# Routing in groups of three tiles, first-half rows from six tiles, scatters between the key copies, and another order of the last tile

## The reference, cut to what matters

```
attn_out = _attn_ref(q, k, v)                     # band of 31 keys and 24 block summaries per query
x = attn_out.transpose(0, 2, 1, 3).reshape(1536, 512)
logits = x @ w_gate
noisy_logits = logits + log1p(exp(x @ w_noise)) * noise
top2 = the two largest of noisy_logits            # of 8 experts
top2_w = softmax over the two
for e in range(8):
    for k in range(2):
        mask = top2[:, k] == e
        h = maximum(x[mask] @ w1[e], 0)
        out[mask] += top2_w[mask, k] * (h @ w2[e])
h = out @ w_in;  r = maximum(h, 0);  result = (s * r * r + b) @ w_out
```

## Time and profile before

| | us |
|---|---|
| median of 3 runs | 706.74 (703.12, 706.74, 707.35) |
| the profiled execution, its own time | 703.65 |
| its span | 702.0 |
| PE busy in the span | 683.7 |
| DVE, ACT, POOL busy | 261.0, 216.1, 309.4 |

### The profile page before, as it was taken

How to read it: one execution, slowest core, us unless ns; L and a number is a source line. 1 busy time by engine, 2 the same in 40 slices (tenths; PEclk the granted TensorE clock), 3 DMA queues, 4 the chain that set the end, 5 groups by cost and what they waited for, 6 DMA issues and landing times.

```text
span 702.0 us, 10455 instructions
## 1 busy us (share of the span) xinstructions
PE 683.7 (97%) x4065; PEld 569.8 (81%) x4065; DVE 261.0 (37%) x551; ACT 216.1 (31%) x499; POOL 309.4 (44%) x278
## 2 busy tenths in 40 slices
PE   8898989999999999999999999999999999999998
PEld 3466789788888888888999899888888888888886
DVE  6467766431230212312121244944505235051330
ACT  2458955221220311203131313411324113141231
POOL 1415745567988396697889562302021020200000
PEclk9999968999999999999999999999999999999999
DMA  9996433699979195792979599932012020100001
GB/s 261 255 289 183 168 136 134 221 397 362 405 258 400 54 388 197 254 382 76 384 249 397 183 336 315 379 113 61 1 60 61 1 60 1 45 15 1 0 1 60
DMA packets 55966, 132.34 MB, mean 189 GB/s; under 512 B 8712, under 2 KB 11016, under 8 KB 55920
## 3 DMA queue, kind: packets, MB, share of 16 engines
q0 software_dynamic: 28144, 82.77, 33.7%
q1 hardware_dynamic: 27155, 47.77, 20.9%
q10 hardware_dynamic: 621, 1.18, 0.7%
HBM read 104.79 MB, written 25.97 MB: 186 GB/s over the span
## 4 chain that ended last, share of the span: by engine, by line
PE 91%; issue 2%; DMA 2%; ACT 2%; DVE 1%; POOL 1%; SPq 0%; POOLq 0%
PE ps L380 27%; PE ps L382 27%; PE ps L381 27%; PE ps L1531 2%; PE ps L1464 1%; PE ps L1419 1%; DMA v_all<-v_all 1%; PE ps L1447 1%; PE ps L1391 1%; ACT prob L693 1%; PE ps L1427 1%; PE ps L1669 1%; PE ps L1456 1%; POOL kwin L567 1%; POOL x_sorted L582 1%
## 5 line engine op out<-in xcount | busy, mean ns | idle before, releaser
L546 POOL TENSOR_TENSOR w_lo<-w_raw,w_hi 128x1024 fp32r<-128x1024 f32 x56 | 134.2, 2416 | 20.5 <-DMA w_hi<-in_w_pieces_dram 19.7
L967 DVE SCALAR_TENSOR_TENSOR h_lo<-ps,h_hi 128x448 fp32r<-128x448 f32 (+2 forms) x64 | 36.7, 574 | 197.2 <-ACT h_hi L704 197.2
L380 PE MATMUL ps<-x_hi,w_hi 128*128 128x448 f32 (+2 forms) x256 | 88.2, 345 | 0.0
L704 ACT ACTIVATE h_hi<-ps 128x448 fp32r<-128x448 f32 (+2 forms) x64 | 32.3, 505 | 181.0 <-PE ps L382 181.0
L381 PE MATMUL ps<-x_lo,w_hi 128*128 128x448 f32 (+2 forms) x256 | 88.0, 344 | 0.0
L382 PE MATMUL ps<-x_hi,w_lo 128*128 128x448 f32 (+2 forms) x256 | 88.0, 344 | 0.0
L380 PE MATMUL ps<-w_hi,h_hi 128*128 128x512 f32 x216 | 86.8, 402 | 0.0
L382 PE MATMUL ps<-w_hi,h_lo 128*128 128x512 f32 x216 | 84.5, 391 | 0.0
L381 PE MATMUL ps<-w_lo,h_hi 128*128 128x512 f32 x216 | 84.5, 391 | 0.0
L1313 DVE SCALAR_TENSOR_TENSOR sqr<-relu,sbb 128x512 f32<-128x512 f32 x48 | 36.2, 754 | 112.9 <-ACT relu L838 112.2
L381 PE MATMUL ps<-y_lo,w_hi 128*128 128x512 f32 (+1 forms) x200 | 76.1, 381 | 0.0
(11 more groups left out here) (228 smaller groups left out, 1125.0 us busy)
## 6 DMA issues: line engine op xcount, KB each, us to landing
w_raw<-in_w_pieces_dram POOLq DMA_DIRECT2D x56, 512.0 KB, 13.8
w_hi<-in_w_pieces_dram POOLq DMA_DIRECT2D x56, 512.0 KB, 15.3
xb<-x_sorted SPq DMA_DIRECT2D x25, 256.0 KB, 7.5
y_sorted<-ysb SPq DMA_DIRECT2D x25, 256.0 KB, 2.0
x_sorted<-zrow SPq DMA_DIRECT2D x7, 896.0 KB, 15.0
w_raw<-in_w_pieces_dram SPq DMA_DIRECT2D x8, 512.0 KB, 4.7
w_hi<-in_w_in_dram POOLq DMA_DIRECT2D x8, 512.0 KB, 7.8
w_raw<-in_w_in_dram SPq DMA_DIRECT2D x8, 512.0 KB, 8.3
```

What stands on the lines that cost most here:

```text
L380: pe.matmul(acc, l_hi, r_hi, start=start, stop=False, skip_group_check=True)
L546: pool.tensor_tensor(piece(w_lo, slot, k), piece(w_raw, slot, k), piece(w_hi, slot, k).bitcast(F32), ALU.subtract).then_inc(pieces_split, 1)
L704: act.activation(hi[:, i // FT % 2, i % FT, 0:rows], ps[:, i % FT, 0:rows], ACT.Relu).then_inc(sg.hhi_ready, 1)
L967: dve.scalar_tensor_tensor(out=lo[:, at, i % FT, 0:rows], in0=ps[:, i % FT, 0:rows], scalar=0.0, in1=hi[:, at, i % FT, 0:rows].bitcast(F32 ...
```

## The change

`GROUP_OF` becomes four groups of three tiles (was 4, 3, 3, 2), so a group's `noise_exp` and `noise_ln` come in slots 3, 6 and 9 (were 4, 7, 10), and its DVE steps one slot earlier too; the last group has three tiles. All ranks stand in bank 7. `EARLY_TILES` is 6. POOL's first 12 scatters are issued one by one between the last key copies, most of them after a wait for a progress count of PE (`pv_done`: values of so many tiles done; `turned`: twice per tile). The last slot of the loop is written out in another order, and in the first head `ranks(3)` moves into the middle of `down_early(0)`.

```diff
-EARLY_TILES = 7
+EARLY_TILES = 6
-GROUP_OF = ((0, 4), (4, 7), (7, 10), (10, 12))
-RANK_BANK = (7, 7, 2, 7)
+GROUP_OF = ((0, 3), (3, 6), (6, 9), (9, 12))
-ROUND_AT = (8, 9, 11)
-GMAX = 4
+ROUND_AT = (8, 10, 11)
+GMAX = 3
@@ POOL
-            key_windows(9)
-            key_windows(10)
             pool.wait_ge(zeros_done, 16)
             pool.wait_ge(pos_ready, 1)
-            for t in range(*GROUP_OF[0]):
-                if t == 2:
-                    key_windows(11)
-                scatter(t)
-            for g in range(1, len(GROUP_OF)):
+            scatter(0, 0)
+            pool.wait_ge(pv_done, 7)
+            scatter(0, 1)
+            key_windows(9)
+            pool.wait_ge(turned, 16)
+            scatter(1, 0)
+            pool.wait_ge(pv_done, 8)
+            scatter(1, 1)
+            key_windows(10)
+            pool.wait_ge(turned, 18)
+            scatter(2, 0)
+            pool.wait_ge(pv_done, 9)
+            scatter(2, 1)
+            pool.wait_ge(pos_ready, 2)
+            scatter(3, 0)
+            key_windows(11)
+            scatter(3, 1)
+            pool.wait_ge(pv_done, 10)
+            scatter(4, 0)
+            pool.wait_ge(scores_done, 12)
+            scatter(4, 1)
+            pool.wait_ge(turned, 22)
+            scatter(5, 0)
+            pool.wait_ge(pv_done, 11)
+            scatter(5, 1)
+            for g in range(2, len(GROUP_OF)):
@@ ACT, first_head
                 noise_exp(last)
+                noise_ln(last)
                 up_early(0)
-                noise_ln(last)
                 up_early(1)
@@ DVE, the loop and behind it
                 if s == NT - 1:
-                    route_top(2)
-                    route_chosen(2)
+                    normalise(s)
                 if s >= 1:
                     read_logits(s - 1)
+                if s in (3, 6, 9):
+                    route_a(s // 3 - 1)
                 if s in (4, 7, 10):
-                    route_a(s // 3 - 1)
-                if s in (5, 8):
                     route_top(s // 3 - 1)
-                if s == 6:
-                    route_c(0)
-                if s == 9:
-                    route_c(1)
+                if s in (5, 8, 11):
+                    route_c(s // 3 - 1)
+                if s == 8:
                     early_count()
-                normalise(s)
-                if s in (5, 8):
+                if s < NT - 1:
+                    normalise(s)
+                if s in (4, 7, 10):
                     route_chosen(s // 3 - 1)
...
-            route_c(2)
             split_first(1)
             read_logits(NT - 1)
             route_a(3)
             up_early(0)
+            up_early(1)
             split_first(2)
-            up_early(1)
             route_top(3)
@@ PE, the loop and behind it
-            for s in range(1, NT):
+            for s in range(1, NT - 1):
...
-                if s == 6:
+                if s == 5:
                     pe.wait_ge(xT_ready, s)
                     ranks(0)
-                if s == 9:
+                if s == 8:
                     pe.wait_ge(xT_ready, s)
                     ranks(1)
                     early_counts()
                 logits(s - 1)
                 values(s)
+            turn_probs(NT - 1)
+            turn_x(NT - 2)
+            values(NT - 1)
+            pe.wait_ge(xT_ready, NT - 1)
             ranks(2)
+            logits(NT - 2)
@@ PE, first_rows and first_part
+                pe.wait_ge(rank_read, 3)
                 turn_x(NT - 1)
...
-                pe.wait_ge(rank_read, 3)
-                down_early(0)
-                pe.wait_ge(lg_ready, NT)
-                ranks(3)
-                pe.matmul(ps[:, 6, 0:E], ones[:, :], before[:, NT, :], start=True, stop=True).then_inc(counts_done, 1)
+                down_early(0, rank_last)      # rank_last: these three steps, after the first of its two row tiles
```

More of the change, by code:

```diff
@@ L578, in spread_means, with scatter @@
                                    ).then_inc(means_in[b][part], 16)
-            def scatter(t):
-                for c in range(2):
-                    pool.indirect_dma_start(out=x_sorted, out_offset=bass.IndirectOffsetOnAxis(pos_i[:, t, c:c + 1], 0),
-                                            in_=x_sb[:, t, :], in_offset=None).then_inc(scattered, 16)
+            def scatter(t, c):
+                pool.indirect_dma_start(out=x_sorted, out_offset=bass.IndirectOffsetOnAxis(pos_i[:, t, c:c + 1], 0),
+                                        in_=x_sb[:, t, :], in_offset=None).then_inc(scattered, 16)
             key_windows(2)
@@ L606, in _ @@
                 for t in range(*GROUP_OF[g]):
-                    scatter(t)
+                    for c in range(2):
+                        scatter(t, c)
             pool.wait_ge(scores_done, NT)
@@ L1055, in route_c @@
                 dve.wait_ge(rank_done, g + 1)
-                rank = ps[:, RANK_BANK[g], L_RANK:L_RANK + n * E].rearrange("p (t e) -> p t e", e=E)
+                rank = ps[:, 7, L_RANK:L_RANK + n * E].rearrange("p (t e) -> p t e", e=E)
                 dve.tensor_tensor(rank_all[:, at:to, :], rank, bc(cst[:, C_ECAP:C_ECAP + E], n, 1), ALU.add).then_inc(rank_read, 1)
@@ L1477, in ranks @@
                 for t in range(at, to):
-                    acc = ps[:, RANK_BANK[g], L_RANK + (t - at) * E:L_RANK + (t - at + 1) * E]
+                    acc = ps[:, 7, L_RANK + (t - at) * E:L_RANK + (t - at + 1) * E]
                     pe.matmul(acc, tri[:, :], chosen[:, t, :], start=True, stop=False)
@@ L1495, in _ @@
             values(0)
-            for s in range(1, NT):
-                if 3 < s + 1 < NT:
+            for s in range(1, NT - 1):
+                if s >= 3:
                     scores(s + 1)
-                if s == 7:
+                if s == 6:
                     pe.wait_ge(rank_read, 1)
-                if s == 10:
+                if s == 9:
                     pe.wait_ge(half_ready, 1)
@@ L1603, in down_early, with rank_last @@
                     down(head, 0, 0, PART, g, between, ha_hi, ha_lo)
+                def rank_last(t):
+                    if t == 1:
+                        pe.wait_ge(lg_ready, NT)
+                        ranks(3)
+                        pe.matmul(ps[:, 6, 0:E], ones[:, :], before[:, NT, :], start=True, stop=True).then_inc(counts_done, 1)
                 up_early(0)
                 up_early(1)
-                pe.wait_ge(rank_read, 3)
-                down_early(0)
-                pe.wait_ge(lg_ready, NT)
-                ranks(3)
-                pe.matmul(ps[:, 6, 0:E], ones[:, :], before[:, NT, :], start=True, stop=True).then_inc(counts_done, 1)
+                down_early(0, rank_last)
                 up_early(2)
```

## The result

The changed kernel took **709.88 us** (median of 22 runs, 704.42 to 718.75), the kernel before 706.34 us beside it (22 runs, 702.24 to 708.78): ratio 1.0055, 95% interval 1.0034 to 1.0076. Forecast were 709 us and "within 1%", so the number and the class held. The same pair was then timed on two more chips, and there the ratio was not the same: 1.0076 [1.0041, 1.0110] where the kernel before takes 703.99 us, but **0.9954 [0.9930, 0.9978]** where it takes 715.99 us. Both things want an explanation: the +3.5 us, which is the sum of the prediction, and the 12 us by which the kernel before is longer on some chips while the changed one is longer by 4 only, of which the prediction knew nothing.

A forecast was written before the change was run, and what follows sets the result against it. PE bounds the kernel, busy 97% of the span; only the chain to the second rows was open. Loop and last tile +0.4, routing +0.8, scatters +2.5 make 3.7 us, added to 705.2: 709 us, own range 706 to 712.

The forecast's parts named there:

- The loop: Attention loop up to tile 11's last exponentials: earlier routing gains against added table loads, sum -0.5 us, bounds -2.3 and +1.75.
- Single scatters among the key copies: POOL's 12 scatters between key copies in the loop: just hidden, cost 0, or up to 1.5 us.
- T: Start of the first head's first product on PE, forecast 0.4 us later, near 103.7 us.
- The last tile: Last exponentials to the first head's first product, at half clock: 12.2 us, 0.9 more; bounds 0 and +1.5.
- Routing of the last group: DVE's chain in the first head until the last group's row numbers are ready: T + 13.0, 0.8 us later.
- The ranks' wait: PE reaches `ranks(3)` in the first head about 0.6 us ahead of DVE's choices and waits, at no further cost.
- Scatters: Last group's scatters on POOL, six instead of four: 2.5 us more before the second rows load.
- The new wait: PE's wait in the first head for the second 256 rows: grows from 1.35 us to 4.0 us.
- Rival 2: PE's clock falls to half in the longer wait for the second rows, costing 2.8 us: 712 us; chance 0.15.
- Rival 3: The last tile keeps full clock, its PE work takes 5 us less: 701.5 us; chance 0.20.
- The forecast case: Every link of the chain to the second rows as summed: 709 us, range 706 to 712; chance 0.50.

The follow-up runs named there:

- b1: The changed kernel run again, unaltered, on a fast chip: 709.37 us, ratio 1.0076 to the kernel before.
- g2: The changed kernel with the third group's noise logarithm replaced by an exponential, so no table loads in the last slots: 711.50 us, ratio 1.0078 to the kernel before.
- b3: The kernel before with scatters of groups 0 and 1 issued singly, each behind a mark of PE's work: 705.66 us, ratio 1.0009.
- b4: b3 plus a new routing order for the last group: `ranks(3)` inside `down_early(0)`, `route_c(3)` ahead of `split_first(3)`: 705.13 us, ratio 1.0006 to the kernel before.
- g1: b4 plus seven useless products ahead of the last tile's turn and eight in the wait for the second rows: 707.38 us, ratio 1.0025 to the kernel before.
- g3: The changed kernel with tile 10's logits ahead of tile 11's values, and DVE's normalisation behind reading the logits: 712.91 us, ratio 1.0070 to the kernel before.
- e1: The kernel before with two more scatters behind the last four, rewriting tile 4's rows, on a slow chip: 719.71 us, ratio 1.0046.
- c1: The changed kernel run again, unaltered, on a slow chip: 713.26 us, ratio 0.9954 to the kernel before.
- b2: The changed kernel with the single scatters of groups 0 and 1 put back into bursts, on a fast chip: 714.47 us, ratio 1.0116 to the kernel before.
- e2: The changed kernel with 16 products of zeros on PE ahead of the wait for the second rows, slow chip: 711.86 us, ratio 0.9942 to the kernel before.
- e3: The kernel before with seven products of zeros on PE ahead of the last tile's turn, slow chip: 716.02 us, ratio 1.0001.
- h1: The kernel before, bursts kept, with the new last-group routing order and seven useless products ahead of the last tile's turn, slow chip: 717.26 us, ratio 1.0045.

## Why the prediction was right, point by point

- **The loop, forecast -0.5 us.** Measured -0.2 (b1) and +1.1 (first execution). The gain (earlier pairs, three tiles in the first group) and the loss (third pair ahead of the last exponentials) both came; g2 sizes the loss at 1.95 us where the prediction had 1.75. The extra of the first execution is one slot: 7.5 us from tile 6's exponentials to tile 7's, against 6.0 in b1, and its half clock from 68.0 to 71.4 us lies in it. A load takes 1.28 us here too, and the exponential behind it starts 0.01 us after its end (97.75). The Trainium skill (ScalarE: Activation LUTs, What ACT_TABLE_LOAD costs) has 2.66 us for every switch, load and drain together. The traces disagree with it for this place: there is no room for a drain in these rows, and two switches less in g2 saved 1.95 us together.
- **Single scatters among the key copies, cost 0.** Right on a fast chip as far as b3 shows it (1.0009 [0.9985, 1.0033]); the 4.8 us of the prediction are 4.7 by its own terms, 2.5 and 2.2. With seven early tiles PE waits 2.2 to 2.4 us for the first rows and T comes 12.4 to 12.6 us behind the exponentials instead of 11.2 (b3, b4, g1).
- **The last tile, forecast +0.9.** +1.0 in the first execution, with half clock through it as the prediction had it, and +0.2 in b1, where the clock is back 1.2 us ahead of T. What the order alone adds is open: g3, which undoes it, takes 0.4 back.
- **Routing of the last group, forecast +0.8 (to T + 13.0).** This step failed: T + 11.7 and T + 10.4, so -0.5 and -1.8. It took the second hidden-value step, at T + 6.3, from the earlier trace rows, where half clock lasts 5.6 us behind T. In the changed kernel half clock lasts 3 us behind T in the first execution and ended 1.2 us ahead of T in b1, and the step ended at T + 5.3 and T + 4.0, for DVE waits there for hidden values that PE makes. g3 is the check: its half clock lasts 5.5 us behind T, and the step ends at T + 6.3, `pos_i` at T + 12.7. The other 0.3 us are in what follows the step, 6.4 us in all three where 6.7 were counted. The ranks' wait of 0.6 us was as forecast (0.56) in the first execution and 0.35 in b1.
- **Scatters, forecast +2.5.** +2.9; e1 alone gives +2.4. The new wait was forecast at 4.0 us and is 4.2 (4.17, 4.20, 4.15 in c1). Mechanism and size hold, though both of its ends came earlier than forecast: the turn at T + 26.4 and T + 25.2 instead of T + 27.3, PE's own work at T + 22.3 and T + 21.0 instead of T + 23.3. Both moved with PE's clock, and the difference kept its size.
- **Rival 2, the clock falls in the new wait, chance 0.15.** This did happen, in every trace of the changed kernel with its wait left as it is (first, b1, c1, b2, g2, g3), and in e1. It costs 1.3 to 1.6 us by the stretch behind the turn and 1.4 by e2, not the 2.8 that the rival gave, because half clock lasts 3.4 us and not 5.6. In g3 it lasts 6.8 us, 133.1 to 139.9, and costs 2.1. The Trainium skill (TensorE: Matmul & The Clock Gate, HAM oscillation) has the array return to the half rate in long enough idle gaps between bursts; by that rule, which I weighed too lightly, this was to be expected, and the traces agree.
- **Rival 3, full clock in the last tile, 0.20.** Not seen as such; b1 has a shorter half clock (10 us) and still no full one. In g2, without the loads, the clock is 1.00 to 100.9 us, 4.4 us behind the last exponentials, and T is no earlier for it (11.4 us behind them, as in b1). The reasoning from 1.59 us of idle time that bring the fall does not hold by itself, as b3 and b4 show. What brings the fall in the last tile stays open.

So the median came out within 1 us in part by luck. A term of +0.8 turned out -0.5 to -1.8, and a clock loss of 1.3 to 1.6 us that the forecast did not count offset it. The forecast case and rival 2 were one case; they had been priced as alternatives. And the two executions stand at +6.2 and +2.5 us against the one trace of the kernel before, so the +3.5 us of the medians, near the forecast +3.7, are not the sum of either.

**What the prediction had no case for** is the slow chip, where the change is 0.5% faster. Shown is this: there the loop of burst forms is 12.8 to 13.1 us longer (e1, e3; h1 57.9 in place of 46.0, 11.9 longer), the long slots are those in which scatters are issued in a row, and the single scatters of c1 and e2 have no such slots, only one of 7.1 us, with a late mark under two scatters in a row. For the kernel before, of which there is no trace on a slow chip, that fits the medians, 715.99 - 703.99 = 12.0. For the changed one 713.26 - 709.37 = 3.9, of which the loop has 1.1; c1 and b1 differ otherwise by the clock in the last tile. All late marks that were found fall under scatters issued in a row or just behind them, yet on a fast chip the same burst of six delays none. Not shown is that the bursts are the cause. Single scatters in the kernel before, which would tell it apart from the groups and rounds, ran on fast chips alone, and so did bursts in the changed kernel. Nor is it shown by what way a scatter could hold back marks that PE sets, or what makes a chip slow. One more trait goes with it, and makes what these traces say of the stall weaker: of the 384 landings of the scatters (24 scatters, 16 each) the traces on fast chips hold 382 to 384, e3's and h1's 184 and 181, e1's 174 of 416, and c1's and e2's 227 and 230. Whether recording itself plays a part in the slow chips' time, no run shows.

## What to carry to other kernels

Sum a chain up to the wait it ends in, then price what that wait does to the clock as a part of the same case: a wait of over 4 us amid dense products cost its length and 1.3 to 2.1 us more, in seven traces of seven. When several engines run by each other's pace, a term taken from a stretch at half clock holds only if that stretch stands at the same place after the change. And time a small change on more than one chip: here the sign of 0.5% depended on it.

## What the runs showed of the hardware

- The same kernel has a median of 704 to 706 us on three sets of runs and 714 to 716 us on two others; in the traces of its forms on the latter, 12 to 13 us more lie in some 25 us of the program, around rows of indirect scatters.
- On the slow chips a mark that PE sets while scatters are issued in a row reaches DVE or ACT late, by 1.7 us (c1) to 6.5 (e3).
- In the first head, half clock followed all waits of 4.0 to 4.4 us, one of 1.9 us (e3) and one of 2.4 us (h1), but neither 1.28 (b3) nor 1.35 us (before), nor e2's wait filled with products.
- Seven products of no use stood ahead of a last tile at full clock in e3 and in h1, on slow chips, and not in g1. The full clock also came without them: at the end of that tile in e1, and from its start in b3 and b4, behind 1.59 us of idle time.
